# Gated-delta attention and two MLPs on one core: two attention blocks merged into one unrolled program, keys read transposed from DRAM

## The reference

```python
k_n = k / (np.linalg.norm(k, axis=-1, keepdims=True) + 1e-06)
for t in range(S):
    y[:, :, t] = q_t @ state
    v_old = state^T k_t
    state = state + beta_t * outer(k_t, v_t - v_old)
...
h = x @ w_in;  g = (a0 + a1 h + a2 h^2 + a3 h^3) / (1 + |b0||h| + |b1|h^2 + 1e-6);  x = g @ w_out
h = x @ w_in2; g = relu(h)^2;                                                    out = g @ w_out2
```

## Time and profile before

| | us |
|---|---|
| median of 3 runs (lowest, highest) | 1212.5 (1211.85, 1216.46) |
| the profiled execution, its own time | 1213.86 |
| its span, first to last instruction | 1212.0 |

### The profile page before, as it was taken

One profiled execution on the slowest core, in us unless ns is written; L12 is line 12 of the kernel. 1 busy time (PEld: TensorE's weight loads), 2 busy tenths in 40 slices (PEclk: granted clock), 3 DMA queues, 4 the chain that ended last, 5 costly groups with the idle time before them and its releaser, 6 DMA issues.

```text
span 1212.0 us, 19944 instructions
## 1 busy us (share of the span) xinstructions
PE 1140.5 (94%) x6480; PEld 984.5 (81%) x6480; DVE 791.8 (65%) x1432; ACT 652.6 (54%) x1310; POOL 520.3 (43%) x649
## 2 busy tenths in 40 slices
PE   6877589999999699999999999989999999999998
PEld 5766578999999587888888888878888888888886
DVE  4799968887444699887888888885434333434332
ACT  6866623333333797877778787865333333333332
POOL 7976743334333397887878788740000000000000
PEclk9978779999999899999999999999999999999999
DMA  7875325344444420101010100324010101001000
GB/s 126 169 138 126 53 63 126 75 98 99 107 86 111 130 66 1 53 1 54 1 53 1 34 19 1 105 92 118 1 53 1 53 1 53 1 8 45 1 26 26
DMA packets 201711, 71.88 MB, mean 59 GB/s; under 512 B 165152, under 2 KB 190880, under 8 KB 201632
## 3 DMA queue, kind: packets, MB, share of 16 engines
q1 hardware_dynamic: 201632, 70.90, 24.4%
HBM read 48.86 MB, written 22.02 MB: 58 GB/s over the span
## 4 chain that ended last, share of the span: by engine, by line
PE 61%; DVE 4%; ACT 1%; issue 1%; ACTq 0%; DVEq 0%
PE ps_y L1079 10%; PE ps_y L1081 10%; PE ps_y L1080 10%; PE ps_h L1064 10%; PE ps_h L1066 10%; PE ps_h L1065 10%; DVE w_in_lo L1198 1%; DVE ps_h L1235 1%; DVE cubic L1213 0%; DVE g_hi L1228 0%; DVE ps_h L1219 0%; DVE w_out_lo L1201 0%; DVE g_lo L1243 0%; ACT w_in_hi L1102 0%; ACT coef L1122 0%
## 5 line engine op out<-in xcount | busy, mean ns | idle before, releaser
L1064 PE MATMUL ps_h<-x_hi,w_in_lo 128*128 128x512 f32 x576 | 226.7, 394 | 14.1 <-DVE g_lo L1243 7.3
L1065 PE MATMUL ps_h<-x_lo,w_in_hi 128*128 128x512 f32 x576 | 226.2, 393 | 0.0
L1066 PE MATMUL ps_h<-x_hi,w_in_hi 128*128 128x512 f32 x576 | 225.9, 392 | 0.0
L1079 PE MATMUL ps_y<-g_hi,w_out_lo 128*128 128x512 f32 x576 | 224.2, 389 | 0.1
L1081 PE MATMUL ps_y<-g_hi,w_out_hi 128*128 128x512 f32 x576 | 224.1, 389 | 0.0
L1080 PE MATMUL ps_y<-g_lo,w_out_hi 128*128 128x512 f32 x576 | 224.1, 389 | 0.0
L1254 DVE TENSOR_TENSOR q<-h_sq 128x512 f32<-128x512 f32 x96 | 66.3, 691 | 135.7 <-ACT h_sq L1143 134.1
L664 POOL TENSOR_TENSOR inv_diag<-inv_rows,own_block 128x128 f32<-128x128 f32 x192 | 85.8, 479 | 157.3 <-PE ps_z L707 128.6
L1064 PEld LDWEIGHTS ps_h<-x_hi,w_in_lo 128*128 128x128 f32 x576 | 109.1, 189 | 38.6 <-DVE g_lo L1243 8.7
L1150 ACT ACTIVATE g_hi<-q 128x512 fp32r<-128x512 f32 x96 | 60.7, 633 | 141.5 <-PE ps_y L1081 137.0
L1323 POOL TENSOR_TENSOR head_times_q<-q,g_hi 128x512 f32<-128x512 f32 x96 | 124.5, 1297 | 11.0 <-DVE g_hi L1228 11.0
(11 more groups left out here) (85 smaller groups left out, 2147.6 us busy)
## 6 DMA issues: line engine op xcount, KB each, us to landing
shared<-w_in SPq DMA_DIRECT2D x32, 192.0 KB, 4.2
shared<-w_out SPq DMA_DIRECT2D x32, 192.0 KB, 4.4
vkp<-k_in SPq DMA_DIRECT2D x12, 384.0 KB, 4.2
ktq<-q_in SPq DMA_DIRECT2D x12, 384.0 KB, 3.9
vkp<-v_in SPq DMA_DIRECT2D x12, 384.0 KB, 4.2
iq<-q_in SPq DMA_DIRECT2D x24, 192.0 KB, 3.1
x_first<-y_t SPq DMA_DIRECT2D x24, 192.0 KB, 2.4
shared<-x_first SPq DMA_DIRECT2D x6, 768.0 KB, 6.0
```

Of the source, the lines that this page charges most:

```text
L1064: pe.matmul(bank(n), lo, x_hi[:, slot, k, :], start=(k == 0), stop=False)
L1065: pe.matmul(bank(n), hi, x_lo[:, slot, k, :], start=False, stop=False)
L1066: mm = pe.matmul(bank(n), hi, x_hi[:, slot, k, :], start=False, stop=(k == KT - 1))
L1079: pe.matmul(ps_y[m][:, :], lo, g_hi[:, d, :], start=(f == 0), stop=False)
```

## The change

The first two blocks become one function `build_attention` without loops and without a barrier between them. Only the first 22 groups (`LEAD`) are prepared before the scan begins; group n + 22 is prepared in step n of the scan, so steps 0 to 25 carry one preparation each.

- The keys are no longer normalised before use. K^T comes from DRAM beside q^T (`kq_in`, on the host put in that layout), so the PE transposes are gone. ACT spreads it (`spread_keys`, two activations for two groups). N needs only 64 columns a pair. The norm is put into `key_beta` = beta/norm^2, into `head_beta`, and into v (`scale_v`, on DVE: v times norm).
- DVE instead of POOL masks the products straight from PSUM (`take_products`), and takes N of the first 16 groups (`take_first_n`); ACT takes N of the others (`take_n`). `new_state` goes from DVE to ACT, as two activations.
- In the scan PE's order is the old one with `products` behind `end_z`. DVE's other work before the scan is `take_first_n` and `take_products` of groups 0 to 7, and the norms (`sums`, then `scales`, nine small instructions each waiting for the one before) of three chunks. In the scan each of groups 28 to 47 has its norms done four at a time.
- PE, DVE and ACT wait for all 21 constants of POOL before their first work (ACT's first `squares` excepted).
- POOL does nothing after it has made the constants. The inverse goes by four DMAs for 4 groups from DRAM into the block-diagonal `inv_diag`, zeroed once.
- The inversion works in one tile, one round after the other: each of its 62 instructions depends on the one before. Round 0 runs whole before the scan, rounds 1 to 5 in steps 0-5, 6-12, 13-20, 21-28 and 29-36.
- Key, value and product tiles become a ring of 32 groups.

The core of the diff:

```diff
-        k_diag = sb("k_diag", [P, 2, PAIRS, 2, D])
-        ktq = sb("ktq", [D2, 2, HP, P + C])
+    RING = 32
+    LEAD = 22
+    BY_DVE = 16
+    BEFORE_INVERSION = 12
...
+    INV_OPS = 2 * BL - 2
+    INV_RING = 3
+    INV_FROM = (None, 0, 6, 13, 21, 29)
+    INV_TO = (None, 6, 13, 21, 29, 37)
+    INV_EARLY = 0
+    NORM_CHUNKS = ((0, 1), (2, 3, 4), (5, 6)) + tuple((h,) for h in range(7, QUADS))
...
+            def load_kq(h):
+                if h >= 2:
+                    sp.wait_ge(np_done, 4 * h - 4)
+                sp.dma_start(kq[:, h % 2], kq_in[:, h]).then_inc(kq_loaded[h % 2], 16)
...
+            def load_inverse(h):
+
+                sp.wait_ge(inv_stored, 16 * (h // 2 + 1))
+                four, g0 = slice(4 * (h % 2), 4 * (h % 2) + 4), 4 * (h % 2)
+                for s in range(SUB):
+                    sp.dma_start(inv_diag[BL * s:BL * s + BL, four, :, BL * s:BL * s + BL],
+                                 inverse_dram[h // 2, g0:g0 + 4, :, s].rearrange("g p j i -> j g p i")
+                                 ).then_inc(loaded[h % 2], 16)
...
+            store_n(2)
+            load_kq(5)
+            store_inverse(0)
+            load_inverse(0)
+            store_n(3)
...
+            pool.memset(cross[:, :, :, :], 0.0).then_inc(const_ready, 1)
+            pool.memset(neg_cross[:, :, :], 0.0).then_inc(const_ready, 1)
+            pool.memset(inv_diag[:, :, :, :], 0.0).then_inc(const_ready, 1)
+            pool.wait_ge(const_ready, 20)
...
+            def products(g):
+
+                pe.wait_ge(k_diag_ready, g // 2 + 1)
+                pe.wait_ge(kq_loaded[g // 4 % 2], 16 * (g // 8 + 1))
+                old = np_before(g)
+                if old >= 0:
+                    pe.wait_ge(p_ready, old + 1)
+                if old >= BY_DVE:
+                    pe.wait_ge(n_ready, old + 1 - BY_DVE)
+                for p in range(PAIRS):
+                    mm = pe.matmul(np_bank(g)[:, p, :].rearrange("r (a c) -> r a c", a=2),
+                                   k_diag[:, g // 2 % 2, g % 2, 2 * p:2 * p + 2].rearrange("r f h t -> r (f h t)"),
+                                   kq[:, g // 4 % 2, :, g % 4 * PAIRS + p, :], start=True, stop=True)
+                mm.then_inc(np_done, 1)
...
+            pe.wait_ge(const_ready, CONSTS)
+            for g in range(LEAD):
+                products(g)
+            for n in range(LAST_MM):
...
+                if n < GROUPS:
+                    end_z(n)
+                if n + LEAD < GROUPS:
+                    products(n + LEAD)
...
+                act.activation(k_diag[:, j % 2, :, :, 0, :], keys, ACT.Copy, scale=own_half[:, 0:1])
+                act.activation(k_diag[:, j % 2, :, :, 1, :], keys, ACT.Copy,
+                               scale=own_half[:, 1:2]).then_inc(k_diag_ready, 1)
...
+            for n in range(LAST_MM):
+                if n + LEAD - 1 < GROUPS:
+                    take_n(n + LEAD - 1)
+                if n < GROUPS:
+                    take_z_first(n)
+                if n >= 2:
+                    new_state(n - 2)
+                if n < GROUPS:
+                    take_cross(n)
+                if n >= 2:
+                    take_y(n - 2)
+                    take_state(n - 2)
+                if n % 2 == 1 and n + LEAD + 1 < GROUPS:
+                    spread_keys((n + LEAD + 1) // 2)
+                for h in range(7, QUADS):
+                    if n == 4 * h - 25:
+                        squares(h)
+                    if n == 4 * h - 24:
+                        roots(norm_chunk(h))
...
+            for g in range(8, BEFORE_INVERSION):
+                take_first_n(g)
+                take_products(g)
+            invert(0, 0, INV_OPS)
+            scale_v(0)
+            for g in range(BEFORE_INVERSION, BY_DVE):
+                take_first_n(g)
+                take_products(g)
+            sums(5)
+            sums(6)
+            scales(2)
+            for g in range(BY_DVE, LEAD):
+                take_products(g)
+            scale_v(1)
+            invert(1, 0, INV_EARLY)
+            for n in range(LAST_MM):
+                for r in range(1, ROUNDS):
+                    if INV_FROM[r] <= n < INV_TO[r]:
+                        now, end = inverted(r, n), inverted(r, n + 1)
+                        invert(r, now, max(end - 2, now))
+                if 1 <= n <= GROUPS:
+                    effective_q(n - 1)
+                for r in range(1, ROUNDS):
+                    if INV_FROM[r] <= n < INV_TO[r]:
+                        now, end = inverted(r, n), inverted(r, n + 1)
+                        invert(r, max(end - 2, now), end)
+                if n < GROUPS:
+                    scale_z(n)
+                if n + LEAD < GROUPS:
+                    take_products(n + LEAD)
+                for h in range(2, QUADS):
+                    if h >= 7 and n == 4 * h - 25:
+                        sums(h)
+                    if h >= 7 and n == 4 * h - 24:
+                        scales(norm_chunk(h))
+                    if n == 4 * h - 6:
+                        scale_v(h)
```

More of the change, by code:

```diff
@@ L13 @@
 AX = mybir.AxisListType
[L18 to L117, removed]
@@ L151, in build_within_chunks @@
+        ident = sb("ident", [P, P])
         before = sb("before", [P, C])
         own_head = sb("own_head", [P, 2])
[L153 to L160, removed]
[L161 removed]
@@ L810, in _ @@
-            act.preload_act_table_set("natural_log_exp_and_others")
-            act.wait_ge(pads_zero, 2)
-            for c in range(CHUNKS):
-                step(c, c, 0, True)
-            with act.Fori(1, BATCH) as b:
-                for c in range(CHUNKS):
-                    step(b * CHUNKS + c, c, b, False)
-            take_y(GROUPS - 2, CHUNKS - 2, BATCH - 1, False)
-            take_state(GROUPS - 2, CHUNKS - 2, BATCH - 1, False)
-            take_y(GROUPS - 1, CHUNKS - 1, BATCH - 1, False)
+                act.activation(state[:, n % 2], ps_s, ACT.Copy).then_inc(s_ready, 1)
@@ new lines, in _ @@
+            act.preload_act_table_set("sqrt_and_others")
+            squares(0)
+            act.wait_ge(const_ready, CONSTS)
+            spread_keys(0)
+            squares(1)
+            roots(0)
+            spread_keys(1)
+            spread_keys(2)
+            spread_keys(3)
+            squares(2)
+            squares(3)
+            squares(4)
+            roots(1)
+            for j in range(4, 9):
+                spread_keys(j)
+            squares(5)
+            squares(6)
+            roots(2)
@@ L858, in step @@
-            def step(n, c, b, first):
-                if not (first and c < 2):
-                    new_state(n - 2, (c - 2) % CHUNKS, b if c >= 2 else b - 1)
-                if not (first and c < 1):
-                    effective_q(n - 1, (c - 1) % CHUNKS, first)
-                scale_z(n, c, first)
-            dve.memset(cross[:, :, :, :], 0.0).then_inc(pads_zero, 1)
-            dve.memset(neg_cross[:, :, :], 0.0).then_inc(pads_zero, 1)
-            dve.wait_ge(scan_inputs.mask_step, scan_inputs.MASKS)
@@ L868, in _, with inverted @@
-            for n in range(PEELED * CHUNKS):
-                step(n, n % CHUNKS, n // CHUNKS, n < CHUNKS)
-                if inversion.EARLY + n < inversion.TOTAL:
-                    inversion.slot(dve, inversion.EARLY + n)
-            with dve.Fori(PEELED, BATCH) as b:
-                for c in range(CHUNKS):
-                    step(b * CHUNKS + c, c, b, False)
-            new_state(GROUPS - 2, CHUNKS - 2, BATCH - 1)
-            effective_q(GROUPS - 1, CHUNKS - 1, False)
+            def inverted(r, n):
+                early = INV_EARLY if r == 1 else 0
+                share = (INV_OPS - early) * (n - INV_FROM[r]) // (INV_TO[r] - INV_FROM[r])
+                return min(max(early + share, early), INV_OPS)
@@ new lines, in _ @@
+            dve.wait_ge(const_ready, CONSTS)
+            sums(0)
+            sums(1)
+            dve.wait_ge(beta_loaded, 16)
+            scales(0)
+            for g in range(8):
+                take_first_n(g)
+                take_products(g)
+            sums(2)
+            sums(3)
+            sums(4)
+            scales(1)
+            for g in range(8, BEFORE_INVERSION):
[3 more added lines that the diff above has]
+            scale_v(0)
```

951 lines of the change are left out of this document (406 added, 545 removed).

## The result

| us | before | after |
|---|---|---|
| median (lowest to highest, 4 runs each) | 1212.17 (1211.55 to 1216.46) | 1171.46 (1171.25 to 1174.96) |
| first matmul of the scan | 152.14 | 89.06 |
| last matmul of the scan | 403.21 | 363.51 |
| first matmul of the MLPs | 406.88 | 367.17 |
| span | 1212.0 | 1169.7 |

A forecast was written before the change was run, and what follows sets the result against it. Before the scan no engine was a clean bound; in it PE bounds. With the scan starting at 83 (was 152.1) and taking 286.6, it ends at 369.6 (was 403.2): 33.6 off the 1212.5 median, 1179 us; range 1158 to 1203.

The forecast's parts named there:

- Start of the scan at 83: Before the scan: its first matmul comes at 83 us in place of 152.1, within 79 to 90.
- 0.90 a group: Before the scan: PE's products, 8 matmuls a group, take 0.90 us, taken from start_z.
- The inverse on its way, 78 to 81: Before the scan: round 0's inverse leaves at about 69 behind load_kq(5) and is back at 78 to 81 us.
- the 85 that the forecast named as a sign of being wrong: Before the scan: the forecast is wrong if the inverse of round 0 lands after 85 us.
- fourth rival: Before the scan: inverse or keys late, SP's waits in a row; start at 100 rather than 83, 1196 us; 6%.
- five terms: Scan steps 0 to 25: 39.3 (0 to 5), 45.5 (6 to 12), 48.8 (13 to 20), 30 (21 to 25), handoffs 4.7 us.
- the handoffs, 4.7: Scan steps 0 to 25: DVE's lateness reaches PE through three handoffs a step at 0.06, 4.7 us.
- DVE's extras: Scan, every fourth step: scale_v 0.9, next sums 0.95, next scales 2.0 us, less any slack.
- return nothing by themselves: Scan: POOL's spreading, new_state on DVE and the barrier go; hidden behind PE in 4.93 us steps, they gain nothing.
- first rival: Inversion on DVE: chained order costs nothing, a round takes 15.6 us, DVE stays below PE; 1155 us; 12%.
- second: Scan steps 0 to 19: DVE and ACT hold each other in every step, 6.75 us each; 1197 us; 18%.
- third: Scan steps 0 to 25: PE's clock falls to a mean of 0.7, 49 us more, slower than before; 1228 us; 8%.

The follow-up runs named there:

- Run 1: Changed kernel plus 152 matmuls nobody reads on PE before the scan, ahead of the products of groups 8, 14 and 18: 1171.34 us, ratio 0.9643.
- run 2: Changed kernel with ACT waiting for 5 constants, DVE for 15, PE for all only from group 8 on: 1169.26 us, ratio 0.9632.
- run 3: Changed kernel with SP's queue before the scan reordered: store_inverse(0) ahead of load_kq(5), store_n(3) ahead of load_inverse(0): 1169.87 us.
- run 4: Changed kernel with the cut constant waits of run 2 and the SP queue order of run 3 together: 1167.94 us, ratio 0.9633.
- run 10: Changed kernel with new_state back on DVE ahead of effective_q, and ACT's copy of y waiting for it: 1194.01 us.
- run 6: Changed kernel with 60 further independent DVE multiplies of the same sizes between the instructions of round 0 of the inversion: 1178.74 us.
- run 7: Changed kernel without three of the four matmul pairs of the products of groups 22 to 47: 1171.33 us.
- run 8: Changed kernel with the multiplies and adds of inversion rounds 1 to 5 cut to one row each, same instruction count: 1168.54 us.
- run 11: Changed kernel with the last two inversion instructions of a step moved from between effective_q and scale_z to behind take_products: 1175.24 us.
- run 5: Changed kernel with the extra matmuls, cut constant waits and new SP queue order together: 1162.06 us, ratio 0.9577.
- run 12: Changed kernel with run 5's edits, keys' load at the head of SP's step, and last two inversion instructions behind take_products: 1158.19 us, ratio 0.9539.

## Why the prediction was right

The cause was forecast rightly, and the amount within 8 us, in part by luck, as two errors cancelled: the lead was 6.1 us longer than forecast and the scan 12.1 shorter. What follows the scan was 2.6 shorter in the profile, which the forecast did not have either.

- **Start of the scan at 83: it was 89.06.** The constants were ready at 15.7 (16.4) and the norms at 21.5 (22). Round 0 began 4.9 us late and took from 45.41 to 68.8, 23.4 against 23.2. The term that was mis-sized is that of the products: the forecast took 0.90 a group at any clock. Groups 0 to 7 took 9.8 against 8 and groups 8 to 11 6.3 against 3.5; the sums and scales between them took 0.7 more than the 7 forecast. ACT's k_diag and a cold PE made it more:
```profile
37.69 8.53 PE L342 MATMUL ps_np<-kq,k_diag 96*128 96x128 f32 x43 [7.05 <-ACT k_diag L461]
```
43 matmuls from 37.69 on in 8.5 us is 0.20 each, 1.6 a group; PE had idled for 7.05 and was granted 0.61 of its clock. Groups 18 to 21 were slower still: 32 matmuls in 7.2 us from 81.90 on, 1.8 a group, at 0.50 from 84.0 to 88.5. The forecast had said that the clock would be down, and charged it only to the scan's first steps. Run 1 takes the cold clock away from group 8 on and finds 83.6. That this is the forecast's 83 is chance in part: for a PE that keeps 2.4 GHz the forecast had 79; round 0 still began 3.6 late in that run, and what follows the round was 3.2 shorter than forecast.
- **The inverse on its way, 78 to 81.** It left SP behind load_kq(5) as forecast, but at 74.66 and not 69; load_inverse was issued from 80.53 on, and its last part, issued at 81.94, took 3.5 to land. That is 85.4, later than the 85 that the forecast named as a sign of being wrong, and still hidden, as PE reached the scan only at 89.06. When the lead got shorter (runs 1 and 2), waits of that queue showed in steps 0 and 1. That is the fourth rival's mechanism; its start at 100 came about nowhere.
- **Steps 0 and 1** took 14.8 together, against 16.3 (twice 5.9 and 4.5 for the cold clock), at a clock of 0.55. In run 3 they took 10.9, so the whole excess over 11.6 went with the low clock. How far SP's order made that clock is open (run 4).
- **Steps 2 to 25** took 147.0: 24 x 5.80 is 139.2, and 7.8 on top. The forecast's five terms come to 168.3 for 26 steps, 16.7 over 26 x 5.83. Here the size was wrong by half, by two terms: the handoffs, 4.7, cost nothing in the steps in which PE has no gap, and DVE's extras were charged nearly in full where only the 12 steps 2 to 6, 8 to 10, 14, 17, 18 and 22 exceed 5.80. In step 22 it is not DVE but the activation table load, 1.28 on ACT at 227.67. PE's 0.90 is exact: steps without a product are 4.90 (step 26, 5.12, is the one clearly above the 4.93 named as a sign of being wrong), those with one and without a wait 5.80.
- **Steps 26 to 47** with the tail took 112.6 against 113.8, and the border to the MLPs 3.66 against 3.7.
- **new_state, POOL and the barrier "return nothing by themselves".** For POOL's spreading and the barrier no run tests it. Wrong for new_state: with DVE so full, run 10 pays 22.5 us for having it there. It is the inversion in one block ahead of effective_q that makes its place matter: with new_state left at that place the rest of the change would have cost these waits. The forecast asked what DVE's 0.55 us cost and not how long PE would wait for it.

The **first rival**, chaining at no cost, is refuted by run 6 and by round 0's 23.4. The **second**, DVE and ACT holding each other in each step, has its mechanism (7.2 us of waits, 17.8 in run 7) but not its size: 6.75 in each of steps 0 to 19 was forecast by it, and the mean of steps 2 to 19 was 6.22. Its price was worked out wrongly too: the sum holds 127.5 us for these steps (39.3, 45.5 and seven eighths of 48.8) and not 117, so the rival's own time is some 1187 and not 1197. The **third**, the clock, stayed out: 1.00 from step 2 on, with PE's longest wait 1.4 us. It was near: in runs 1, 8 and 11, with PE waiting 1.8 to 3.1 us for z in step 8, the clock of that step was 0.82 to 0.84. The forecast's argument against it, gaps under 1 us in the old scan, doesn't hold: turn_state waited up to 1.5 there. Its price isn't right either: 5.83 us at 0.7 of the clock is 8.3, 2.5 more a step and not 1.9.

A late load of the keys makes step 8 last 6.7 to 7.7 us in some kernels and 9.5 to 10.5 in others. The profiles tell them apart: in runs 1, 8 and 11 PE's wait for z in that step was 1.8 to 3.1 us, the clock was 0.82 to 0.84, and PE's matmuls took 7.4 to 7.7; where it waited 0.7 to 1.7 (the changed kernel and runs 2 to 7 among them) the clock stayed at 1.00 and they took 6.0 or less. Run 10 lies between: with a wait of 2.1 its clock fell only in step 9, to 0.89.

Open: why the MLPs take 806.2 in one execution and up to 809.4 in another; what SP's order is worth in the usual execution; what the loop costs with ACT's z ahead of N; and how much another `LEAD` would give, as no run varies it or takes the merging back.

## What to carry to other kernels

An engine that works in order costs others its latency, not its busy share: before an instruction is put on an engine, look at what stands ahead of it there when its input arrives (0.55 us of work cost 22). When a lead is shortened, follow the gain to the end of the next stage: cuts of 5.5 and 4.0 us in the lead were 2.4 and 3.6 at the scan's end, as waits in the DMA queue and a lower clock took the rest. An edit on one engine can also hold the queue: two instructions moved on DVE made a load 2.4 us late, and one step 3.6 us longer. And where two engines are both near the step's time, taking work from one gives little: 16 us off PE gave 1.6.

## What the runs showed of the hardware

- **A VectorE instruction held by GpSimd.** In run 2 one of DVE's smallest instructions took 3.13 us (3.37, 2.14 and 2.69 in runs 4, 5 and 12); the same one takes 0.18 in the changed kernel. It ended with a GpSimd instruction that ran beside it:
```profile
12.21 3.43 POOL L327 TENSOR_TENSOR iq<-ident 96x1536 f32<-96x1536 f32 x1
...
12.55 3.13 DVE L572 TENSOR_SCALAR norm_work<-root 128x32 f32<-128x32 f32 x1 [0.37 <-ACT root L451]
```
The Trainium skill ("SBUF — State Buffer", Who interferes with whom) says that the two share a pair of ports under an exclusive lock; the trace agrees. Part of the early start of run 2 was lost to it.
- **A matmul nobody reads can pay.** 152 of them in PE's idle time brought 4.8 us at the scan's start, 3.0 at its end in the profiles and 5.9 in the medians (run 5 against run 4, whose profile is its fastest execution), as the products behind them then ran at 2.4 GHz. From 30 us to the scan's start the granted clock was 0.97 in run 5 and 0.61 in run 4.
- **A chained DVE instruction** of 240 elements starts 0.44 after the one it depends on, an independent one 0.32 (run 6).
